# Phase angles: the middle channel tile as stacked split halves, after the fp32 products and the transposes

## The reference, cut to what matters

```python
theta = x @ w_theta                     # x: output of the first layer, w_theta: 192 x 192
zr, zi = x * np.cos(theta), x * np.sin(theta)
y = einsum('ts,bsd->btd', w_tok_r, zr) + einsum('ts,bsd->btd', w_tok_i, zi)   # 4224 x 4224 each
u = x + y
return u + np.maximum(u @ w_ch, 0.0)
```

## Time and profile before

| | |
|---|---|
| median of 3 runs | 2716.61 us (2715.55 to 2717.97) |
| the profiled execution's own time | 2715.52 us |
| its span, first to last instruction | 2713.7 us |
| TensorE busy | 2701.2 us, 13983 matmuls |
| VectorE busy | 2121.6 us |
| ScalarE busy | 1048.6 us |

### The profile page before, as it was taken

How to read it: one execution, slowest core, us unless ns; L and a number is a source line. 1 busy time by engine, 2 the same in 40 slices (tenths; PEclk the granted TensorE clock), 3 DMA queues, 4 the chain that set the end, 5 groups by cost and what they waited for, 6 DMA issues and landing times.

```text
span 2713.7 us, 34681 instructions
## 1 busy us (share of the span) xinstructions
PE 2701.2 (100%) x13983; PEld 2489.1 (92%) x13983; DVE 2121.6 (78%) x2353; ACT 1048.6 (39%) x1366; POOL 218.4 (8%) x272
## 2 busy tenths in 40 slices
PE   8999999999999999999999999999999999999999
PEld 7999999999999999999999999999999998888888
DVE  7878887888789788788888887997766885665655
ACT  6543433333333333333333333333322563433333
POOL 0111001001011011011010010010110210000000
PEclk9999999999999999999999999999999999999999
DMA  6979678678677687697696786776873210000000
GB/s 209 212 176 228 169 206 197 157 208 200 171 204 181 181 201 179 184 224 163 181 209 160 201 202 173 203 177 175 200 192 112 59 36 25 25 35 32 31 36 32
DMA packets 106063, 416.89 MB, mean 154 GB/s; under 512 B 11344, under 2 KB 32816, under 8 KB 105904
## 3 DMA queue, kind: packets, MB, share of 16 engines
q0 software_dynamic: 35200, 155.73, 32.5%
q1 hardware_dynamic: 70704, 258.95, 27.3%
HBM read 371.38 MB, written 38.93 MB: 151 GB/s over the span
## 4 chain that ended last, share of the span: by engine, by line
PE 98%; DVE 1%; ACT 0%; issue 0%; DMA 0%; DVEq 0%; SPq 0%; ACTq 0%
PE bank L1369 24%; PE bank L1370 24%; PE bank L1371 24%; PE bank L1464 2%; PE bank L1468 2%; PE bank L1466 2%; PE bank L1465 2%; PE bank L1467 2%; PE bank L1485 2%; PE bank L1483 2%; PE bank L1484 2%; PE bank L1490 2%; PE bank L1489 2%; PE bank L1315 2%; PE bank L1385 1%; PE bank L1321 1%
## 5 line engine op out<-in xcount | busy, mean ns | idle before, releaser
L1369 PE MATMUL bank<-w_h,z_op 128*128 128x448 f32 (+1 forms) x3465 | 1232.1, 356 | 2.0 <-DVE z_op L1010 1.2
L1371 PE MATMUL bank<-w_h,z_op 128*128 128x448 f32 (+1 forms) x3465 | 1226.5, 354 | 0.0
L1370 PE MATMUL bank<-w_l,z_op 128*128 128x448 f32 (+1 forms) x3465 | 1226.3, 354 | 0.0
L645 ACT ACTIVATE w_h<-w_raw 128x1344 fp32r<-128x1344 f32 (+1 forms) x385 | 486.2, 1263 | 1063.4 <-PE bank L1371 913.4
L1369 PEld LDWEIGHTS bank<-w_h,z_op 128*128 128x128 f32 x3465 | 650.9, 188 | 44.1 <-issue 2.0
L1371 PEld LDWEIGHTS bank<-w_h,z_op 128*128 128x128 f32 x3465 | 650.8, 188 | 41.3
L1370 PEld LDWEIGHTS bank<-w_l,z_op 128*128 128x128 f32 x3465 | 651.0, 188 | 40.2
L1022 DVE TENSOR_TENSOR w_l<-w_raw,w_h 128x1344 fp32r<-128x1344 f32 (+1 forms) x385 | 567.6, 1474 | 61.8 <-ACT w_h L645 61.1
L606 POOL DMA_DIRECT2D w_raw<-in_w_tok x220 | 193.3, 901 | 1857.7 <-DVE w_l L1022 1119.1
L1243 DVE SCALAR_TENSOR_TENSOR hid_l<-bank,hid_h 128x472 fp32r<-128x472 f32 (+1 forms) x216 | 139.8, 647 | 184.5 <-ACT hid_h L886 182.8
L1058 DVE TENSOR_TENSOR Y<-Y,bank 128x1344 f32<-128x1344 f32 (+1 forms) x105 | 154.7, 1473 | 103.6 <-PE bank L1371 102.6
(11 more groups left out here) (149 smaller groups left out, 2797.7 us busy)
## 6 DMA issues: line engine op xcount, KB each, us to landing
w_raw<-in_w_tok SPq DMA_DIRECT2D x220, 672.0 KB, 4.5
w_raw<-in_w_tok POOLq DMA_DIRECT2D x220, 672.0 KB, 6.9
z_raw<-z_out SPq DMA_DIRECT2D x85, 576.0 KB, 6.7
z_out<-zf SPq DMA_DIRECT2D x65, 384.0 KB, 6.5
x_win<-in_xin SPq DMA_DIRECT2D x22, 585.0 KB, 6.3
out<-res SPq DMA_DIRECT2D x16, 708.0 KB, 3.1
ends<-u_l POOLq DMA_DIRECT2D x44, 96.0 KB, 2.2
v_raw<-in_v SPq DMA_DIRECT2D x9, 177.0 KB, 3.7
```

Of the source, the lines that this page charges most:

```text
L645: nc.scalar.activation(w_h[:, s % WRING, :, 0:n], w_raw[:, SLOT[s], :, 0:n], ACT.Copy).then_inc(wh_ready, 1)
L1369: mm(to, zh, wh, start=(k == 0 and not goes_on), stop=False, skip_group_check=goes_on)
L1370: mm(to, zh, wl, start=False, stop=False, skip_group_check=goes_on)
L1371: last = mm(to, zl, wh, start=False, stop=(k == KC - 1), skip_group_check=goes_on)
```

## The change: what it does

For groups 1 to 21 (63 units) the fp32 product of the middle tile is replaced. ScalarE copies rows 0 to 63 of a unit's middle tile, rounded to fp32r, into `mids[0:64, ., 0]`, and rows 64 to 127 into `mids[64:128, ., 1]` (`share_hi`). VectorE subtracts these from the tile and writes the rest into the other 64 partitions (`share_lo`). So `mids[:, ., e]` holds 64 channels of one batch twice, high part and rest stacked. `theta_twice` holds the matching 64 rows of the weights twice, split once at the start into `theta_h` and `theta_l`. Two matmuls of 192 columns per batch then give all the products: four fp32r matmuls of 192 columns for one fp32 product of 384. They come after the two outer fp32 products and the three transposes, and the last of them raises `theta_ready`. Group 0 keeps the fp32 product, with weights of its own (`theta_mid`). The halves are made one stage ahead for r = 0 and two stages ahead for r = 1 and 2. For n >= 8 the products of unit r = 1 come one stage sooner, and with them its store.

```diff
+def share_stage(n, r):
+    return theta_stage(n, r) - (1 if r == 0 else 2)
 def product_stage(n, r):
-    return theta_stage(n, r) + (1 if n in EARLY else 3)
+    return theta_stage(n, r) + (1 if n in EARLY else 2 if n >= 8 and r == 1 else 3)
...
-        theta_w = sb(prep, "theta_w", [P, 4 * D])
+        theta_w = sb(prep, "theta_w", [P, 2 * D])
+        theta_h = sb(prep, "theta_h", [P, 2 * D], F32R)
+        theta_l = sb(prep, "theta_l", [P, 2 * D], F32R)
+        mids = sb(prep, "mids", [P, 2, 2, P], F32R)
...
             sp.dma_start(theta_w[:], w_theta).then_inc(const_loaded, 16)
+            sp.dma_start(theta_mid[:], w_theta_mid).then_inc(mid_loaded, 16)
             load_w(0)
             load_w(1)
             load_x(1)
+            sp.dma_start(theta_twice[:], w_theta_twice).then_inc(twice_loaded, 16)
             load_w(2)
...
+            def share_hi(n, r):
+                m, src = KC * n + r, (attn_1 if n == 1 else attn)
+                act.wait_ge(conv_tap, conv_done(n))
+                if m >= KC + 2:
+                    act.wait_ge(theta_ready, m - 1)
+                for e, rows in enumerate((slice(0, 64), slice(64, P))):
+                    nc.scalar.activation(mids[rows, m % 2, e], src[rows, 1, r * P:(r + 1) * P],
+                                         ACT.Copy).then_inc(shared_hi, 1)
...
             for r in range(KC):
                 piece_hi(1, r)
+            act.wait_ge(twice_loaded, 16)
+            nc.scalar.activation(theta_h[:], theta_twice[:], ACT.Copy).then_inc(theta_hi, 1)
...
                 for n in range(1, GP):
                     for r in range(KC):
+                        if share_stage(n, r) == s:
+                            share_hi(n, r)
                         if theta_stage(n, r) == s:
                             turn(KC * n + r)
...
+            def share_lo(n, r):
+                m, src = KC * n + r, (attn_1 if n == 1 else attn)
+                for e, (rows, other) in enumerate(((slice(0, 64), slice(64, P)), (slice(64, P), slice(0, 64)))):
+                    dve.wait_ge(shared_hi, 2 * (m - KC) + e + 1)
+                    vec.tensor_tensor(mids[other, m % 2, e], src[rows, 1, r * P:(r + 1) * P],
+                                      mids[rows, m % 2, e].bitcast(F32), ALU.subtract).then_inc(shared_lo, 1)
...
             for r in range(KC):
                 piece_lo(1, r)
+            dve.wait_ge(theta_hi, 1)
+            vec.tensor_tensor(theta_l[:], theta_twice[:], theta_h[:].bitcast(F32), ALU.subtract).then_inc(theta_lo, 1)
...
                 if s + 2 < NS:
                     w_lo(s + 2)
+                for n in range(1, GP):
+                    for r in range(KC):
+                        if share_stage(n, r) == s:
+                            share_lo(n, r)
...
-                mm(angle_bank, src[:, 1, rows], theta_w[:, D:3 * D], start=True, stop=False)
-                mm(angle_bank[:, 0:D], src[:, 0, rows], theta_w[:, 0:D], start=False, stop=False)
                 if n == 0:
+                    mm(angle_bank, src[:, 1, rows], theta_mid[:], start=True, stop=False)
+                    mm(angle_bank[:, 0:D], src[:, 0, rows], theta_w[:, 0:D], start=False, stop=False)
                     pe.wait_ge(attn_ready, 1)
-                mm(angle_bank[:, D:GW], src[:, 2, rows], theta_w[:, 3 * D:4 * D], start=False, stop=True)
+                    mm(angle_bank[:, D:GW], src[:, 2, rows], theta_w[:, D:2 * D], start=False, stop=True)
+                else:
+                    mm(angle_bank[:, 0:D], src[:, 0, rows], theta_w[:, 0:D], start=True, stop=True)
+                    mm(angle_bank[:, D:GW], src[:, 2, rows], theta_w[:, D:2 * D], start=False, stop=True,
+                       skip_group_check=True)
                 for t in range(TP):
                     last = nc.tensor.transpose(x[:, t * P:(t + 1) * P], src[:, t, rows], ident[:])
+                if n:
+                    if m == KC:
+                        pe.wait_ge(theta_lo, 1)
+                    pe.wait_ge(shared_lo, 2 * (m - KC + 1))
+                    for e, cols in enumerate((slice(0, D), slice(D, 2 * D))):
+                        both = mids[:, m % 2, e]
+                        mm(angle_bank[:, cols], both, theta_h[:, cols], start=False, stop=False, skip_group_check=True)
+                        last = mm(angle_bank[:, cols], both, theta_l[:, cols], start=False, stop=True,
+                                  skip_group_check=True)
                 last.then_inc(theta_ready, 1)
```

More of the change, by code:

```diff
@@ L269, in at, with build @@
     return i * per + const
-def build(nc, w_tok, xin, taps_w, w_theta, w_ch, u, v3, w1, w2, ident_in, spread_in, z_out, out):
+def build(nc, w_tok, xin, taps_w, w_theta, w_theta_mid, w_theta_twice, w_ch, u, v3, w1, w2, ident_in, spread_in, z_out, out):
     top = ExitStack()
@@ L305, in build @@
             diag_0 = sb(first, "diag_0", [P, TAPS, P])
-            sb(first, "to_w_l", [P, WRING * KC * TW - TAPS * P])
+            theta_mid = sb(first, "theta_mid", [P, 2 * D])
+            sb(first, "to_w_l", [P, WRING * KC * TW - TAPS * P - 2 * D])
             diag_1 = sb(first, "diag_1", [P, TAPS, P])
+            theta_twice = sb(first, "theta_twice", [P, 2 * D])
             diag = (diag_0, diag_1)
@@ L350, in build @@
             with ExitStack() as first:
+                sb(first, "to_ends_1", [P, 1000])
                 ends_1 = sb(first, "ends_1", [P, 2, GW], F32R)
@@ L371, in build @@
         const_loaded = sem("const_loaded")
+        mid_loaded = sem("mid_loaded")
+        twice_loaded = sem("twice_loaded")
+        theta_hi = sem("theta_hi")
+        theta_lo = sem("theta_lo")
+        shared_hi = sem("shared_hi")
+        shared_lo = sem("shared_lo")
         ident_loaded = sem("ident_loaded")
@@ L1020, in w_lo @@
                 dve.wait_ge(wh_ready, s + 1)
+                if s == WRING - 1:
+                    dve.wait_ge(theta_lo, 1)
                 n = width(STAGES[s][2])
@@ L1336, in _ @@
             pe.wait_ge(const_loaded, 16)
+            pe.wait_ge(mid_loaded, 16)
             for r in range(KC):
@@ L1551 @@
     th = twice(moe_w_theta)
-    theta = np.concatenate([th[0:P, 0:D], th[P:2 * P], th[2 * P:, D:]], axis=1)
+    theta = np.concatenate([th[0:P, 0:D], th[2 * P:, D:]], axis=1)
+    theta_twice = np.concatenate([np.concatenate([moe_w_theta[P:D]] * 2), np.concatenate([moe_w_theta[0:64]] * 2)], axis=1)
     ch = twice(moe_w_ch)
@@ L1562 @@
     w2 = moe2_w_ch2.reshape(FT, P, D).transpose(1, 0, 2)
-    arrays = dict(w_tok=w.reshape(CHUNKS, TG, 4, P, KC * TW), xin=win, taps_w=taps, w_theta=theta, w_ch=ch,
+    arrays = dict(w_tok=w.reshape(CHUNKS, TG, 4, P, KC * TW), xin=win, taps_w=taps, w_theta=theta, w_theta_mid=th[P:2 * P],
+                  w_theta_twice=theta_twice, w_ch=ch,
                   u=u, v3=v3, w1=w1, w2=w2, ident=np.eye(P, dtype=x.dtype),
```

## The result

The changed kernel takes 2705.2 us (2704.95 to 2705.75, 6 runs) against 2715.98 us for the kernel before in the same comparison: 10.8 us less, ratio 0.996 with a 95% interval of 0.9947 to 0.9973. The forecast was 2704.0. The profiled execution's span is 2703.3 us, 10.4 us less than the 2713.7 before.

What follows compares the result with a forecast made beforehand. TensorE's stream of starts was taken as the bound. Saving 13.2 us over 63 units less a 0.6 us stall gives -12.6 us: 2715.5 becomes 2702.9, and 1.1 us for the median gives 2704.0 us; range 2698 to 2711.

Steps and rivals of the forecast that it cites:

- The bound: Whole kernel: time is the sum of TensorE's starts, busy 2701.2 of 2713.7 us; what leaves its stream is gained fully.
- What is removed: Middle tile's fp32 product of 384 columns leaves TensorE's stream: 0.65 us in each of 63 units, 41.0 us.
- What is added: Four fp32r matmuls of 192 columns per unit on TensorE: 0.11 us each, 0.44 us a unit; net saving 13.2 us.
- the two lower bounds: Price of a 192-column fp32r matmul: 0.094 us by columns, 0.11 us by its weight load; the larger was taken.
- column-paced rival: New matmuls cost 0.094 us each because the weight load hides better: 17.3 us gained less 0.6, 2699.9 us; chance 0.12.
- the floor at 0.147 us: New matmuls run no faster than 320-column ones: 3.9 us gained less 0.6, 2713.3 us; chance 0.06.
- the fp32 rate: Narrow fp32r matmuls take 0.325 us each, 0.65 us more a unit than what they replace: 2758 us; chance 0.09.
- VectorE and ScalarE: Splitting adds 0.57 us a unit on VectorE and 0.62 on ScalarE, 36 and 39 us in all, costing no time.
- The moved products: Mid-kernel, r = 1 products one stage sooner: 2.7 us left before their banks' next use, so the move costs nothing.
- Late halves: TensorE stalls about 0.6 us once, in group 2; rival: all 21 r = 0 units wait, about 2716 us, chance 0.07.
- The start: Kernel start: splitting the weights adds 0.52 us on ScalarE and 0.55 on VectorE, under 4.2 us of cover; costs nothing.
- Sum: Whole kernel: -13.2 + 0.6 = -12.6 us; 2702.9 us for a run like the profiled one, 2704.0 us as median.

Runs made afterwards that it cites:

- the runs with 96 and 384 columns: Changed kernel with each unit's four 192-column matmuls cut into eight of 96 columns, 2733.0 us; or made two of 384 columns, computation altered, 2698.8 us.

## Why the prediction was right, point by point

- **The bound.** TensorE's stream sets the time before and after. Shown: removing four matmuls a unit gives back 26.8 of the 28.2 us of their starts.
- **What is removed.** 0.65 us a unit as read; 0.644 to the nanosecond.
- **What is added.** Four intervals of 0.11 us. Measured 0.110 to 0.112, four of them and the hand-over 0.45. So 0.195 us a unit instead of 0.21, 12.3 us instead of 13.2. The choice between the two lower bounds was the step that mattered, and the runs with 96 and 384 columns settle it against the columns. That the 0.11 us is the load's own time rests on the loads behind a pause, 0.11 us for 128 columns and 0.055 for 64. The column-paced rival (2699.9), the floor at 0.147 us (2713.3) and the fp32 rate (2758) are out. The Trainium skill's page "TensorE: Matmul & The Clock Gate", section "LDWEIGHTS (loading the stationary operand)", gives the columns over 1.2 as the load's nanoseconds, 107 at 128; the trace agrees with its 110. The sustained 81 ns at N=128 that the same page of the Trainium skill gives (section "Back-to-back issue gap") does not hold here, where 96 columns take 110.
- **VectorE and ScalarE.** 287 and 303 ns an operation against 285 and 310 predicted, and VectorE at 86%: right. Free: right but for the waits at the halves, and only with the moved products.
- **The moved products.** Here one step was incomplete. "Moving the products alone thus costs nothing; the unit after it waits for them with more room, not less" is true, and the move alone measures as nothing. What the prediction did not ask is what the splits would do if the products stayed: with 0.39 us of room before the unit and 0.6 us of new work in front, 4 us would have gone back. The number stood because the change had the move in it, not because a step of the prediction asked for it.
- **Late halves.** 0.6 us once, in group 2, was the forecast. It was 0.45 there, and groups 7 and 3 added 0.37 and 0.15. The mechanism and the place were right; the other two were looked at too coarsely.
- **The start.** Costs nothing: the mix begins at 21.51 us in both. The rest of stage 2's weights ends at 31.5 instead of 30.84, and stage 2 starts at 35.09 in both.
- **Sum.** The profiled spans differ by 10.4 us against 12.6 forecast: 0.9 from the unit, 0.4 from the halves, 0.8 from the pace of the mix in that execution and 0.1 of other gaps. The forecast is nearer to the measured time (1.2 us) than to the measured gain (10.8 against 12.6), and that is luck: the kernel before came out at 2715.98 in this comparison and not at the 2716.6 that the forecast was counted from.

## What to carry to other kernels

A narrow matmul with a stationary operand of its own costs 0.11 us here, at 96 columns as at 192, so count loads and not columns once the moving side is short; one product of 384 columns (0.17 us) is cheaper than two of 192 (0.22). Work put on an engine with room to spare is free only up to the next deadline in its queue: look at each place for the microseconds between its end and the wait that it feeds. Put what arrives late at the end of the unit that uses it, and look at what else has to move ahead when a split is put in.

## What the runs showed of the hardware that was not expected

- Matmuls that each load a 128 x 128 fp32r operand start 0.11 us apart whether they have 96 or 192 columns; at 320 columns (0.147 us) and 384 (0.173 us) the pace follows the columns.
- The mix's 448-column matmuls have two paces, 0.203 and 0.207 us, each held for whole stages. The slower one appears in 13 stages of the changed kernel's profiled execution, in 5 of the same kernel's second one, in 1 of the kernel before, in 3 of that with only the move, and in none of the fourteen profiles behind stage 92. The granted clock is full in all of them. The cause is open; between these executions it is worth up to 1.8 us.
- The changed kernel's second profiled execution had waits of 0.4 and 1.2 us at 231 and 238 us. ScalarE and then VectorE had waited for a weight block; VectorE works without a pause from 224.72 us until the operand that TensorE waits for is ready, at 237.72:

```profile
223.36 1.33 ACT L663 ACTIVATE w_h<-w_raw 128x1344 fp32r<-128x1344 f32 x1 [2.63 <-DMA w_raw<-in_w_tok]
224.72 1.56 DVE L1062 TENSOR_TENSOR w_l<-w_raw,w_h 128x1344 fp32r<-128x1344 f32 x1 [3.23 <-ACT w_h L663]
...
237.78 0.48 PE L1429 MATMUL bank<-w_h,z_op 128*128 128x448 f32 x1 [1.04 <-DVE z_op L1054]
```

  In the first profiled execution ScalarE waited for that block 0.66 us instead of 2.63, and TensorE had no wait there. So the time at which a transfer in the first chunks lands differs between executions of one kernel, and here it cost 1.6 us; how much of the kernel's spread (2704.57 to 2708.51 us) it makes is not shown.
